# The slots of the second weight buffer, 4112 instead of 4096 bytes apart

## The reference

```python
kv = np.einsum('bhsd,bhse->bhde', k, v)            # q, k, v: 8 x 8 x 576 x 64
out = np.einsum('bhsd,bhde->bhse', q, kv)
rms = np.sqrt(np.mean(out * out, axis=-1, keepdims=True) + 1e-06)
x = out / rms * g_norm                             # then reshaped to 4608 x 512

gate = 1.0 / (1.0 + np.exp(-(x @ w_gate)))         # 512 x 1536
val = x @ w_val                                    # 512 x 1536
x = (gate * val) @ moe_w_out                       # 1536 x 512

h = x @ w_in                                       # 512 x 2048
g = np.where(h > 0.0, h, np.exp(np.minimum(h, 0.0)) - 1.0)
y = g @ moe2_w_out                                 # 2048 x 512
```

## Time and profile before

| | |
|---|---|
| median of 2 runs | 1836.8 us (1834.77 and 1838.83) |
| the profiled execution: its time | 1837.31 us |
| its span, from the first instruction to the last | 1835.5 us |
| mean granted TensorE clock | 0.997 of full |
| PE busy | 1807.7 us (98%), 8304 matmuls |
| PEld busy | 1504.7 us (82%), 8304 weight loads |
| DVE, ACT, POOL busy | 741.7, 387.8, 81.9 us |
| instructions | 21760 |

### The profile page before, as it was taken

The page is one execution under the profiler, slowest core; times in us unless marked ns, Lnnn a source line. Parts: engine busy times, 40 slices in busy tenths (PEclk is TensorE's granted clock), DMA queues, the critical chain, the costliest instruction groups (busy, mean ns, idle before and its releaser), DMA issues.

```text
span 1835.5 us, 21760 instructions
## 1 busy us (share of the span) xinstructions
PE 1807.7 (98%) x8304; PEld 1504.7 (82%) x8304; DVE 741.7 (40%) x1240; ACT 387.8 (21%) x710; POOL 81.9 (4%) x117
## 2 busy tenths in 40 slices
PE   7998999999999999999999999999999999999999
PEld 6887888888888888888888888888888888888887
DVE  3676532222222222212222376454545454444443
ACT  6784310101111010101010232121212121211111
POOL 3552000000000000000000000000000000000000
PEclk9999999999999999999999999999999999999999
DMA  9895420000101010101010132010101010101000
GB/s 235 246 277 184 131 75 1 32 14 2 44 0 46 0 46 0 46 0 46 0 46 0 59 124 69 1 46 0 46 0 46 0 46 0 46 0 46 1 22 23
DMA packets 69792, 93.74 MB, mean 51 GB/s; under 512 B 4736, under 2 KB 43648, under 8 KB 69760
## 3 DMA queue, kind: packets, MB, share of 16 engines
q1 hardware_dynamic: 69232, 92.29, 16.6%
q10 hardware_dynamic: 528, 1.05, 0.2%
HBM read 65.01 MB, written 28.31 MB: 51 GB/s over the span
## 4 chain that ended last, share of the span: by engine, by line
PE 90%; DMA 1%; DVE 1%; issue 0%; ACT 0%; POOL 0%; SPq 0%; POOLq 0%; ACTq 0%; DVEq 0%
PE bank L470 53%; PE bank L487 37%; DMA qkv<-in_k_dram 0%; DMA w_raw<-in_moe_w_in_dram 0%; DVE o L681 0%; ACT y L627 0%; POOL sq L393 0%; PE bank L420 0%; DMA x_gated<-y 0%; DMA out_dram<-y 0%; PE bank L438 0%; PE bank L429 0%; DVE w_pre L701 0%; DVE x_hl L695 0%; PE bank L439 0%
## 5 line engine op out<-in xcount | busy, mean ns | idle before, releaser
L470 PE MATMUL bank<-x_hl,w_rest 128*128 128x512 f32 x3024 | 713.2, 389 | 0.0
L470 PEld LDWEIGHTS bank<-x_hl,w_rest 128*128 128x128 f32 x3024 | 567.8, 188 | 117.7
L487 PE MATMUL bank<-w_rest,u_hl 128*128 128x512 f32 x1620 | 386.3, 389 | 0.8 <-DVE u_hl L712 0.8
L487 PEld LDWEIGHTS bank<-w_rest,u_hl 128*128 128x128 f32 x1620 | 304.0, 188 | 64.2 <-issue 1.2
L719 DVE TENSOR_TENSOR u_f<-bank,act_f 128x512 f32<-128x512 f32 x108 | 74.7, 691 | 618.9 <-PE bank L470 618.9
L470 PE MATMUL bank<-x_hl,w_pre 128*128 128x512 f32 x1296 | 302.3, 389 | 2.0 <-DVE x_hl L695 1.3
L470 PEld LDWEIGHTS bank<-x_hl,w_pre 128*128 128x128 f32 x1296 | 243.0, 188 | 53.4 <-DVE x_hl L695 2.2
L487 PE MATMUL bank<-u_hl,w_rest 128*128 128x512 f32 x1188 | 282.4, 389 | 0.0
L487 PEld LDWEIGHTS bank<-u_hl,w_rest 128*128 128x128 f32 x1188 | 223.0, 188 | 46.2
L613 ACT ACTIVATE act_f<-act_f 128x512 f32<-128x512 f32 x144 | 91.0, 632 | 591.8 <-DVE act_f L733 591.8
L733 DVE TENSOR_SCALAR act_f<-bank 128x512 f32<-128x512 f32 x144 | 99.4, 690 | 270.4 <-PE bank L470 270.4
(11 more groups left out here) (50 smaller groups left out, 666.2 us busy)
## 6 DMA issues: line engine op xcount, KB each, us to landing
qkv<-in_q_dram SPq DMA_DIRECT2D x32, 288.0 KB, 5.2
qkv<-in_k_dram SPq DMA_DIRECT2D x32, 288.0 KB, 5.7
qkv<-in_v_dram SPq DMA_DIRECT2D x32, 288.0 KB, 6.1
x_attention<-o SPq DMA_DIRECT2D x32, 288.0 KB, 3.6
x_gated<-y SPq DMA_DIRECT2D x36, 256.0 KB, 2.0
x_raw<-x_gated SPq DMA_DIRECT2D x9, 1024.0 KB, 5.2
out_dram<-y SPq DMA_DIRECT2D x36, 256.0 KB, 2.0
x_raw<-x_attention SPq DMA_DIRECT2D x8, 1024.0 KB, 5.2
```

The lines of the kernel that those rows point to most:

```text
L470: mm = pe.matmul(dst[:, :], w[:, a, m * P:(m + 1) * P], x_hl[:, m, b, :], start=(m == 0 and a == b == 0), stop=(m == KT - 1 and a == 1))
L487: mm = pe.matmul(ACC[m][:, :], lhs, rhs, start=(j == 0 and a == b == 0), stop=(j == tiles - 1 and a == 1))
```

## The change

A slot of `w_rest` gets 4 float32 elements (16 bytes) of room that nothing uses, and `slot(n)` leaves them out. The 29 slots then start 4112 bytes apart: slot number i of the buffer lies 16 i bytes further than before, 0 to 448. The buffer is 29 x 16 = 464 bytes longer, and `y` behind it moves by 464 bytes. `w_pre` and all that is declared before `w_rest` stay where they are. No instruction is added, removed or moved, and each reads and writes as many bytes as before, contiguous as before.

```diff
-        w_rest = sb("w_rest", [P, 3 * J1 - PRE, 2, NT], F32R)
+        SKEW = 4
+        w_rest = sb("w_rest", [P, 3 * J1 - PRE, 2 * NT + SKEW], F32R)
...
             if n in PRE_SLOTS:
                 return w_pre[:, PRE_SLOTS.index(n)]
-            return w_rest[:, n - sum(m < n for m in PRE_SLOTS)]
+            return w_rest[:, n - sum(m < n for m in PRE_SLOTS), 0:2 * NT].rearrange("p (a c) -> p a c", a=2)
```

## The result

The changed kernel takes 1869.13 us (median of 2 runs, 1867.27 and 1870.99) against 1836.8 us: ratio 1.0176, 95% interval [1.0111, 1.0241]. A second measurement, with 4 runs of the changed kernel and 11 of the kernel before, gave 1871.0 against 1837.83 us, 1.0180 [1.0163, 1.0197]. I had forecast no difference and a range up to 1846 us.

A forecast was written before the change was run, and what follows sets the result against it. PE, by the distance between matmul starts, was taken to bound the kernel. All terms were taken as zero: 1835.5 + 0 us for the span, a predicted median of 1836.8 us, range 1829 to 1846 us.

The forecast's parts named there:

- What bounds the kernel: PE busy in 98% of the span; dense layers set by 226.67 ns between matmul starts, 1664.6 of 1835.5 us.
- First reason: In `product` and `add_hidden`, pieces at unlike offsets within a slot all take 226.67 ns, so no collision with period 1024 bytes or more.
- Second reason: In attention, six offsets that are no multiple of 512 bytes carry the same 13 ns, so no collision at shorter periods.
- Third reason: The fixed cost is 13.3 ns beside 2048 moving bytes and 12.9 beside 1152, so it doesn't grow with the reads' overlap.
- 5832 matmuls x 0: Matmuls with an operand in `w_rest`, times the change of the distance between starts, taken as zero.
- The uncovered starts: Starts off multiples of 64 bytes, which no trace row shows: 21 of 29 slots, 4212 matmuls, taken as zero.
- A displaced start may lengthen a load by up to 38.9 ns and cost nothing: For 3024 displaced loaded slots, PEld's idle time per load covers a longer load; taken as zero.
- the term of the moving slots: In 1188 matmuls moving a displaced slot, one more 64-byte piece costs 6.7 ns: 7.9 us, range only, forecast zero.
- The rule of the Trainium skill: PE has two read ports, for moving operand and weight load, and never waits on anyone: no collision to remove.
- `y`, the splits, the stores: Splits writing displaced slots, 7 us if a tenth slower, and stores from moved `y`, 0.4 us: both taken as zero.
- B: Lines 470 and 487, slots with i not a multiple of 4: another read step, 13.3 ns, 56 us slower, 1893 us; chance 0.02.
- The sign of being wrong: The prediction is wrong if the distance between matmul starts moves by 8.7 ns in the displaced slots.

The follow-up runs named there:

- experiment 5: Matmul-only program, no kernel layers, varying columns moved, columns loaded, their step and the shift: 512 columns 226.7 ns at shift 0, 233.3 at 32 bytes; 288 columns 131.7 and 133.3.
- experiment 2: Kernel before the change with only `y` moved, by an unused buffer ahead of it, slots still 4096 bytes apart: 1839.46 against 1837.91 us.
- experiment 4: Kernel before the change with 32 unused bytes ahead of `w_pre`, moving all dense-layer buffers alike: 1837.48 against 1837.91 us.
- 3: Kernel before the change with the whole of `w_rest` shifted by 32 bytes, slots still 4096 bytes apart: 1881.11 against 1837.91 us.
- 7: Kernel before the change with the whole of `w_rest` shifted by 256 bytes, slots still 4096 bytes apart: 1838.12 against 1838.26 us.
- 1: Matmul-only program, no kernel layers, with loaded slot, moving tile or both shifted: loaded slot 226.7 ns at 0, 16 and 240 bytes, up to 234.6 elsewhere.
- 9: The changed kernel measured again, against the kernel before on the same chip: 1871.0 us, 33.2 us over it.
- 12: Kernel before the change with three slots in a row sharing a shift, the next three 256 bytes further, up to 2304: 1839.21 against 1838.72 us.

## Why the prediction was wrong, point by point

- **What bounds the kernel: right.** The distance of matmuls sets the dense layers, and the whole 32.0 us came in through it, at the same clock and with the same waits.
- **First reason (offsets within a slot, periods of 1024 bytes and more): right, and blind.** All these offsets are multiples of 512, so of 256.
- **Second reason (attention has six other offsets, and "they carry the same 13 ns"): this step failed.** It took 288-column matmuls as witnesses for 512-column ones. By experiment 5 a shift of 32 to 128 bytes moves a 288-column matmul from 131.7 to 133.3 ns, and a 512-column one from 226.7 to 233.3 (232.5 at 128). The six offsets of attention are 64, 128 and 192 modulo 256, and the 132.9 ns that I read the earlier trace rows lie between the 131.7 and 133.3 that 288 columns take there: the short matmuls were displaced, and hardly paid for it; the trace of before had no 512-column fp32r matmul off a multiple of 256.
- **Third reason (a cost alike for 2048 and 1152 moving bytes is a fixed step): wrong by the same comparison.** It set aligned long matmuls against displaced short ones. With the two fell the term that rested on them: 5832 matmuls x 0, which measured 30.5 us.
- **The uncovered starts: drawn at the wrong line.** I held multiples of 64 bytes for shown. Slots 4, 8, 12, 20, 24 and 28 (64, 128 or 192 modulo 256) cost as well; slots 16 and 17, when loaded, cost next to nothing (226.7 and 227.5 ns). In all 5832 matmuls the mean is (21.4 + 9.1) us / 5832 = 5.2 ns.
- **"A displaced start may lengthen a load by up to 38.9 ns and cost nothing": the cover was no cover.** The load stayed at 188 ns. What grew is the distance, also where only the loaded piece was displaced, by 6.67 ns at most places: 21.4 us where I had taken zero. Only 9.1 us are the term of the moving slots, for which I had kept 7.9. That the two lie near each other is luck: the 6.7 ns came from one more piece of 64 bytes, and the runs show no step at 64.
- **The rule of the Trainium skill** (page "SBUF — State Buffer", section "Who interferes with whom") that PE never waits on anyone and has a read port for each operand, which I set beside the equal distances, doesn't carry as far as I used it: the runs show the distance of two fp32r matmuls changing by 6.67 ns with nothing but the relative place of the two operands. The measurement decides.
- **`y`, the splits, the stores: right,** all unchanged (experiment 2).
- **The rivals.** B was the right side, with its place (lines 470 and 487) and half its price (6.67, not 13.3 ns), but its condition, the start against 64 bytes, was wrong: experiment 4 moves all starts by 32 bytes for nothing. Its chance of 0.02 and the range's upper end rested on the two steps that failed. The change stayed under the 2% to which I gave 0.94, but not for my reason: it is 32 us above the forecast and 23 above the range.
- **The sign of being wrong, 8.7 ns in the displaced slots: too coarse.** No slot moved so far; a mean of 5.2 ns in all 5832 matmuls was enough.

**Shown:** the dependence on the relative place modulo 256 bytes, by constants in the kernel (3, 4, 7), the size of the change in sum, though not for each slot (1, 9), and that unlike offsets are harmless if they are multiples of 256 (12). **Open:** what stalls inside. That the two reads meet in the same part of the memory fits the period and fits that the place counts relative to the other read, but the simple form of it, in which fewer loaded columns cost less, fell in experiment 5, and no run took the load away altogether.

## What to carry to other kernels

Keep the operands of fp32r matmuls with 512 moved and 128 loaded columns at multiples of 256 bytes from each other, and the moving one at a multiple of 32; 16 bytes of room behind each slot cost 1.8% here. Other shapes have other best places (experiment 5) and want their own measurement. And when a trace's rows stand in for a case that it doesn't hold, check that they agree in size too: a short matmul said nothing of a long one.

## What the runs showed that I had not expected

- fp32r with 512 columns takes 226.67 ns at its best places, 233.33 at most others and up to 240.0 (moving start 20 bytes off); bf16 takes 215.8 ns at every shift of the loaded piece that was tried.
- Aligned places are not best at every length: 256 columns take 120.0 ns aligned and 117.8 ns at 64 or 192 bytes, 448 columns 202.6 and 200.0 ns at 0 and 192 bytes.
- The distance has a memory: 272 bytes gave 226.67 or 233.33 ns, depending on the setting before, and `w_pre` matmuls behind displaced slots ran at up to 236 ns for a few matmuls before they were back at 226.67.
- Loading fewer columns does not make the matmul stream faster: 230.0 ns with 64 loaded columns against 226.67 with 128, at shift 0.
